# A convolution's last pair: sum on VectorE in the buffer of x1, the neighbour's transform in other banks, the last transform stored in two parts

## What is computed

```python
# 1: convolution with 7 taps and weights per token and head
w = softmax(weight_gen)                       # (B, S, 8, 7)
out = einsum('bshk,bskhg->bshg', w, x_unf)    # the 7 last tokens, 24 channels per head
# 2: real part of a Fourier transform over tokens and channels, then an MLP
mixed = real(fft(fft(x, axis=1), axis=2))
u = x + mixed
x = u + relu(norm(u) @ w_ch1) @ w_ch2
# 3: rotation, product over all tokens, MLP
theta = x @ w_theta
y = w_tok_r @ (x * cos(theta)) + w_tok_i @ (x * sin(theta))
u = x + y
result = u + relu(u @ w_ch)
```

## Time and profile before

| | |
|---|---|
| median of 3 runs | 3148.22 us (3147.73 to 3152.39) |
| profiled execution, its own time | 3150.33 us |
| its span, first to last instruction | 3148.5 us |
| TensorE busy | 3039.9 us, 97% |
| VectorE, GpSimd, ScalarE busy | 2445.8, 1635.5, 1323.5 us |
| mean granted TensorE clock | 0.989 |
| end of the convolution's last product | 318.8 us |
| first matmul of the third transform | 329.46 us |

### The profile page before, as it was taken

How to read it: one execution, slowest core, us unless ns; L and a number is a source line. 1 busy time by engine, 2 the same in 40 slices (tenths; PEclk the granted TensorE clock), 3 DMA queues, 4 the chain that set the end, 5 groups by cost and what they waited for, 6 DMA issues and landing times.

```text
span 3148.5 us, 57324 instructions
## 1 busy us (share of the span) xinstructions
PE 3039.9 (97%) x17542; PEld 2873.3 (91%) x17542; DVE 2445.8 (78%) x4263; ACT 1323.5 (42%) x2474; POOL 1635.5 (52%) x1536
## 2 busy tenths in 40 slices
PE   6888889999999899999999999999999999999999
PEld 4666469989898899999999999999999999999999
DVE  8887667777778787878878787887878787887776
ACT  2222346666666443433334333433433343333443
POOL 7897026766667554545445453545545454543221
PEclk9999999999999999999999999999999999999999
DMA  7775742332333666666666565665656666565442
GB/s 246 272 279 194 263 148 101 113 115 101 116 111 121 218 228 218 237 216 226 228 219 233 204 241 208 229 237 212 234 205 238 217 231 224 221 230 172 133 150 65
DMA packets 213450, 618.45 MB, mean 196 GB/s; under 512 B 20288, under 2 KB 61504, under 8 KB 211200
## 3 DMA queue, kind: packets, MB, share of 16 engines
q1 hardware_dynamic: 203600, 603.19, 53.9%
q10 hardware_dynamic: 9696, 13.37, 1.5%
HBM read 399.82 MB, written 216.66 MB: 196 GB/s over the span
## 4 chain that ended last, share of the span: by engine, by line
PE 84%; POOLq 6%; DVE 3%; issue 2%; DMA 1%; POOL 1%; SPq 1%; ACT 1%; DVEq 0%; ACTq 0%
PE banks L1657 63%; PE banks L1485 11%; POOLq L1078 6%; PE banks L1595 4%; PE banks L1597 3%; PE banks L1581 2%; POOL head L1076 1%; PE banks L1734 1%; DMA m_scr<-mst 1%; DVE zl L835 0%; DVE hl L810 0%; SPq L467 0%; PE banks L1571 0%; DVE wl L830 0%; PE banks L1573 0%
## 5 line engine op out<-in xcount | busy, mean ns | idle before, releaser
L1657 PE MATMUL banks<-zh,wh 128*128 128x384 f32 x3828 | 1286.9, 336 | 13.3 <-DVE rbuf L887 13.3
L1657 PE MATMUL banks<-zh,wl 128*128 128x384 f32 x3828 | 1280.7, 335 | 0.0
L1657 PE MATMUL banks<-zl,wh 128*128 128x384 f32 x3828 | 1280.5, 334 | 0.0
L887 DVE TENSOR_TENSOR rbuf<-rbuf,banks 128x384 f32<-128x384 f32 x1168 | 646.2, 553 | 312.1 <-PE banks L1657 274.2
L1657 PEld LDWEIGHTS banks<-zh,wh 128*128 128x128 f32 x3828 | 719.9, 188 | 14.5 <-DVE wl L830 7.3
L1657 PEld LDWEIGHTS banks<-zl,wh 128*128 128x128 f32 x3828 | 719.9, 188 | 0.0
L1657 PEld LDWEIGHTS banks<-zh,wl 128*128 128x128 f32 x3828 | 719.5, 188 | 0.0
L1111 POOL TENSOR_TENSOR wsum<-wraw 128x384 f32<-128x384 f32 x176 | 179.6, 1021 | 1021.0 <-DVE wl L830 895.8
L1302 ACT ACTIVATE wh<-wsum 128x384 fp32r<-128x384 f32 x704 | 370.8, 527 | 722.9 <-PE banks L1657 701.5
L1302 ACT ACTIVATE wh<-wraw 128x384 fp32r<-128x384 f32 x528 | 278.5, 528 | 492.8 <-PE banks L1657 492.8
L830 DVE TENSOR_TENSOR wl<-wsum,wh 128x384 fp32r<-128x384 f32 x664 | 446.0, 672 | 34.3 <-ACT wh L1302 5.1
(11 more groups left out here) (147 smaller groups left out, 4276.7 us busy)
## 6 DMA issues: line engine op xcount, KB each, us to landing
wraw<-w_pairs SPq DMA_DIRECT2D x176, 768.0 KB, 6.7
rbuf<-y_scr SPq DMA_DIRECT2D x176, 768.0 KB, 5.7
y_scr<-rbuf SPq DMA_DIRECT2D x160, 768.0 KB, 4.0
xin<-x_pad SPq DMA_DIRECT2D x22, 1728.0 KB, 8.1
z_scr<-zsc SPq DMA_DIRECT2D x33, 768.0 KB, 4.1
zraw<-z_scr SPq DMA_DIRECT2D x33, 768.0 KB, 7.2
x_scr<-x1s SPq DMA_DIRECT2D x22, 576.0 KB, 3.0
t_scr<-tst ACTq DMA_DIRECT2D x44, 288.0 KB, 4.3
```

What stands on the lines that cost most here:

```text
L887: dve.tensor_tensor(part, part, dst(k, i), ALU.add).then_inc(r_done, 1)
L1657: last = pe.matmul(dst, l[w][:, q, :], r[par][:, operand, q, :], start=starts and q == 0 and t == 0, stop=q == 2 and t == 2, skip_group_ch ...
```

## The change

1. `head_taps` of the last pair are 1, 2 and 3, so GpSimd makes one add more. VectorE makes five taps, adds tap 6 to tap 5's buffer, makes the last tap (4), adds that sum to it, and then writes `head[1]` plus the sum straight into `x1s[1]`, in the order (j, b) of that buffer, once GpSimd's three adds, the store of the old `x1s[1]`, dft_seq(9,1) and the eviction of (10,0) are done. The 12 matmuls and the eviction of that pair go away, and the tail's three adds become two plus the one into `x1s[1]`.
2. dft_seq(10,0) writes banks 3 to 5 and waits for no eviction of dft_chan(9,1). dft_seq(10,1) waits for that eviction.
3. dft_chan(10,1) signals after its second block too, and ScalarE evicts and stores its blocks 0 and 1 first and then block 2, with two DMAs each. The weights' conversion comes after all of them. Counts of waits are set to fit.

```diff
@@ head_taps
-            return (1, 2) if final(g, h) else HEAD_TAPS[h]
+            return (1, 2, 3) if final(g, h) else HEAD_TAPS[h]
@@ SyncE
             for h in range(2):
-                sp.wait_ge(t_out[h], 32 * NG)
+                sp.wait_ge(t_out[h], 32 * (NG + h))
@@ VectorE
-            convolve(NG - 1, 1, None)
+            for k in TAP_ORDER[1][:5]:
+                weigh(NG - 1, 1, k)
             dve.drain()
             dve.tensor_tensor(tap[4][:], tap[4][:], tap[5][:], ALU.add)
-            dve.tensor_tensor(tap[2][:], tap[2][:], tap[3][:], ALU.add)
+            weigh(NG - 1, 1, TAP_ORDER[1][5])
             dve.drain()
-            dve.tensor_tensor(tap[4][:], tap[4][:], tap[2][:], ALU.add).then_inc(tail_ready, 1)
-            dve.wait_ge(sum_ready, 2 * NG)
+            dve.tensor_tensor(tap[3][:], tap[3][:], tap[4][:], ALU.add)
+            dve.drain()
+            dve.wait_ge(taps_added, heads(NG - 1, 1) + 3)
+            dve.wait_ge(x1_out[1], 16 * (NG - 1))
+            dve.wait_ge(s_ready, 2 * NG - 2)
+            dve.wait_ge(x1_ready, 2 * NG - 1)
+            dve.tensor_tensor(x1s[1][:].rearrange("p j (b d) -> p b j d", b=2), head[1][:], tap[3][:],
+                              ALU.add).then_inc(x1_ready, 1)
+            dve.wait_ge(sum_ready, 2 * NG - 1)
+            dve.drain()
             for s in range(4):
                 if s == 2:
-                    dve.wait_ge(t_ready, 2 * NG)
+                    dve.wait_ge(t_ready, 2 * NG + 1)
@@ ScalarE
-            def evac_a(g, h):
+            def evac_a(g, h, first=0):
                 act.wait_ge(s_ready, 2 * g + h + 1)
-                act.activation(a1[h][:], banks[:, 0:3, 0:3 * P], ACT.Copy).then_inc(a_ready, 1)
+                act.activation(a1[h][:], banks[:, first:first + 3, 0:3 * P], ACT.Copy).then_inc(a_ready, 1)
@@
-            evac_a(NG - 1, 0)
-            evac_x(NG - 1, 1)
+            evac_a(NG - 1, 0, 3)
             evac_a(NG - 1, 1)
             evac_t(NG - 1, 0, 3)
-            evac_t(NG - 1, 1)
+            act.wait_ge(t_out[1], 32 * (NG - 1))
+            for n, (j0, j1) in enumerate(((0, 2), (2, 3))):
+                act.wait_ge(t_ready, 2 * NG + n)
+                act.activation(tst[1][:, j0:j1].rearrange("p j b d -> p j (b d)"), banks[:, j0:j1, 0:2 * D],
+                               ACT.Copy).then_inc(t_evac, 1)
+                act.drain()
+                for w in range(2):
+                    act.dma_start(t_scr[w, 3 * (NG - 1) + j0:3 * (NG - 1) + j1, :, BH:2 * BH].rearrange("j i x -> i j x"),
+                                  tst[1][P // 2 * w:P // 2 * w + P // 2, j0:j1].rearrange("p j b d -> p j (b d)")
+                                  ).then_inc(t_out[1], 16)
@@ TensorE
-            def dft_seq(g, h):
+            def dft_seq(g, h, first=0):
                 q = 2 * g + h
                 pe.wait_ge(x1_ready, q + 1)
                 if final(g, h):
-                    pe.wait_ge(a_ready, q)
-                else:
+                    pe.wait_ge(t_evac, q - 1)
+                elif not first:
                     wait(pe, t_evac, q)
@@ dft_chan, behind block j
+                    if final(g, h) and j == 1:
+                        last.then_inc(t_ready, 1)
@@
-            dft_seq(NG - 1, 0)
-            pe.wait_ge(x1_ready, 2 * NG - 1)
-            pe.wait_ge(taps_added, heads(NG - 1, 1) + 2)
-            for j in range(3):
-                add_part(head[1], j, True, False)
-            pe.wait_ge(tail_ready, tails(NG - 1, 1) + 1)
-            for j in range(3):
-                last = add_part(tap[4], j, False, True)
-            last.then_inc(sum_ready, 1)
+            dft_seq(NG - 1, 0, 3)
             dft_seq(NG - 1, 1)
             dft_chan(NG - 1, 0, 3)
             dft_chan(NG - 1, 1)
```

More of the change, by code:

```diff
@@ L1517, in dft_seq @@
                     for i in range(3):
-                        last = pe.matmul(bank[i][:, P * j:P * j + P], x1s[h][:, j, P * i:P * i + P], fs[:],
+                        last = pe.matmul(bank[first + i][:, P * j:P * j + P], x1s[h][:, j, P * i:P * i + P], fs[:],
                                          start=True, stop=True)
```

## The result

| | before | changed |
|---|---|---|
| median, 20 runs each on the same chips | 3149.43 us (3147.50 to 3152.59) | 3155.19 us (3152.28 to 3158.14) |
| ratio, 95% interval | | 1.0017 [1.0011, 1.0024] |
| profiled execution, its span | 3150.33, 3148.5 us | 3152.28, 3150.4 us |

The change makes the kernel slower by 0.17%, 5.8 us, where 4.6 us less was forecast. That is less than the 0.2% that the prediction calls no change, but it lies outside its range of 3141.0 to 3146.8 us, and on the other side, and the interval leaves no doubt of the direction. The profiled execution of the changed kernel is the fastest of its twenty.

A forecast was written before the change was run, and what follows sets the result against it. VectorE's end of quarter 3 of the third transform, held by weight conversion, counts: weights 4.2 us earlier plus 0.4 makes 4.6, so 3143.6 us from the median 3148.22; range 3141.0 to 3146.8.

The forecast's parts named there:

- The end of the convolution: Last pair's sum to third transform: x1 add ends near 304.2, weights 4.2 us earlier, SyncE's first store 4.6 us earlier.
- The turns of VectorE and GpSimd: In the last pair's sum, VectorE's SBUF adds and GpSimd's adds hold each other off; x1s 1.15 us later than without.
- the prediction's own rule: A VectorE add with both inputs in SBUF and a GpSimd add take turns; each loses what is left of the other.
- Part 2 at no gain: dft_seq(10,0) in banks 3 to 5 ends about 1.5 us earlier, but that alone brings nothing to the end.
- The split's cost on ScalarE: Storing the last transform in two parts adds about 1.6 us of ScalarE work and gets 1.3 back.
- The prediction's 1.6 less 1.3: ScalarE's added work from the two-part store, about 1.6 us, less 1.3 for part one starting before the last block is done.
- the 0.6 of the expectation: Expectation of the run stored whole: weight conversions start and quarter 3 ends 0.6 us earlier against the x1 add.
- TensorE's start to be of no effect: TensorE starts the third transform 4.9 to 6.2 us earlier, but nothing follows, since the weights hold VectorE.
- The later stages are bound by TensorE and keep the shift: Behind the third transform, the 4.6 us lead of SyncE's queue lasts to the kernel's end.
- The fourth: Rival: stage B's some seven rounds lengthen from 3.87 to 5.23 us, costing 9.5 us, giving 3153.1 us; chance 0.04.

The follow-up runs named there:

- N = 13: Changed kernel plus 13 instructions of already-met waits in TensorE's list behind the last dft_chan; 3144.65 us, ratio 0.9979 to the kernel before.
- 26: Changed kernel plus 26 instructions of already-met waits in TensorE's list behind the last dft_chan; 3146.08 us, ratio 0.9987 to the kernel before.
- N = 3: Changed kernel plus 3 instructions of already-met waits in TensorE's list behind the last dft_chan; 3155.06 us, ratio 1.0018 to the kernel before.
- 200: Changed kernel plus 200 instructions of already-met waits in TensorE's list behind the last dft_chan; 3153.95 us, one run.
- stored whole: Kernel N = 13 with the last transform stored whole instead of in two parts; 3145.40 us, ratio 0.9986 to the kernel before.
- without the third add: Kernel N = 13 with tap 3, GpSimd's third add, left out of the last pair's sum; x1 add ends 10.90 us after GpSimd's end of pair (10,0).
- 230: Kernel before plus 230 instructions of already-met waits in TensorE's list behind its last dft_chan; 3168.83 us, ratio 1.0062 to the kernel before.

## Why the prediction was wrong, point by point

- **The end of the convolution** was right. Forecast and measured, the first two as us behind the head: end of the first four products and the add, 299.1 - 292.3 = 6.8, measured 6.6; end of the x1 add 11.9, measured 11.94; weights 4.2 earlier, measured 4.0 without the run's own 0.42; the last parts' evictions 0.82 and 0.50, measured 0.81 and 0.49; SyncE's first store 4.6 earlier, measured 4.76. VectorE does four quarters in a row at 0.92 each, 0.94 in the sum. TensorE starts the third transform 5.1 earlier, within the 4.9 to 6.2, and as forecast nothing follows from it in this kernel.
- **The turns of VectorE and GpSimd** were right, and their detail nearly. The second add took 2.37 and GpSimd's third 3.59 instead of 2.63. By the prediction's own rule that third add ends at 301.7 and not at the 301.55 of its sum; it ended at 300.98, 301.4 with the run's own 0.42 added. The first add was not held up: GpSimd's second add ended at 297.23, close enough to its start at 297.13.
- **Part 2 at no gain** was wrong by 0.7 us, since I looked at the eviction ahead of dft_seq(10,0) and not at the one that frees the banks behind it.
- **The split's cost on ScalarE** was 0.55 us. The prediction's 1.6 less 1.3 is 0.3; the 0.6 of the expectation came out right by luck, since its own terms add up to 0.14. Its worth was missed altogether, because I took TensorE's start to be of no effect. It has one wherever its low clock lasts past the first quarters.
- **"The later stages are bound by TensorE and keep the shift"** is the step that failed. It took TensorE's list as work only, and put at nothing what moving the loop in the code does. The 26 instructions that went moved the MLP loop's start to six places ahead of a block's end, and each of its two jumps then cost 4.4 and 5.6 us more. No rival had this. The fourth, rounds of stage B getting longer, forecast a slower kernel, but stage B took 79.3 us from SyncE's first store to TensorE's last product of it, and 81.4 before. The trace of before showed what to ask: the gap of 1.27 us at the jump, its releaser "issue", and the row of instruction packets on the page.
- **The rest** agrees: with the layout put right (N = 13 and 26) the change gives 0.9979 and 0.9987, 5.1 and 3.6 us less, where 4.6 was forecast. That the time agrees this closely is in part luck, as the next paragraph shows.

What stays open: stage B's length scatters from 79.3 to 83.9 us between profiles of kernels that don't differ in it, and I found no rule in that. Between 900 and 1500 us of the span five of the profiles (N = 3, 26 and 200, stored whole, without the third add) lose 1.8 to 2.3 us against the kernel before, the others 0.8 or less; this wasn't followed up. Each is more than the single parts are worth, so the worth of each part rests on the timelines and not on the times. How long the clock stays low behind a stop isn't explained either: 3.4 and 6.8 us at the two jumps of the changed kernel, 6.8 at all four jumps with N = 3 and 230, where the jumps take 11.0 to 12.0 us.

## What to carry to other kernels

Any edit of an engine's list ahead of a loop moves the loop in its code, and so can cost or give microseconds far from the edit. Where a result doesn't fit, set the two traces' product starts side by side from the end and look where the difference steps; if it steps at a loop's jump with the releaser "issue", look for packets of the instruction queue there, add a few met waits where that engine is idle and measure again. Compare variants with the list's length held, or the layout is measured along with them. And where two engines are late within a microsecond of each other, freeing one is worth the distance between them and no more.

## What the runs showed of the hardware

- At a jump back of this loop TensorE stands for 1.1 to 1.8 us with the next block's end far off, and for 2.7 to 3.2 us more with it six instructions behind the target; the granted clock falls to its lower level with that, which brings the loss to 4.4 to 5.8 us a jump, and with it three behind the target to 5.8 and 6.7. With 26 instructions in between it stands for 0.9 and 1.3 us more and the clock stays up; with 62 there is no second stop. The product that ends a stop starts 2.2 to 3.1 us after a packet of the instruction queue began.
- 230 instructions that only hold met waits took 25 us on TensorE's sequencer, 0.106 us apart, more than twice what I had taken.
- A VectorE add of two SBUF inputs, 1.36 us, took 2.37 beside a GpSimd add, and that one 3.59 instead of 2.63. Each lost about what the other still had to do: 1.01 us where GpSimd had 1.15 left, 0.96 where VectorE had 1.10 left. The Trainium skill has it so (SBUF — State Buffer, Who interferes with whom): two SBUF inputs on VectorE contend with GpSimd's reads, and the shared ports are locked for one at a time.
- Behind 10 us of idle, TensorE's granted clock stayed at the lower level until 3.2 us after its start in one profile and until 5.9 and 6.1 in two others of nearly the same list. That decides which engine bounds the third transform.
